# Three small operations of the expert stage in another order: a raw copy, its rounding, its low part

## The reference, cut to what matters

```python
for e in range(E):                                  # 4 experts, head width 64
    q = x @ wq[e]; k = x @ wk[e]; v = x @ wv[e]
    scores = scale * (q @ k.transpose(0, 2, 1))     # 576 x 576, causal
    a = np.exp(scores - scores.max(-1, keepdims=True))
    a /= a.sum(-1, keepdims=True) + 1e-09
    ye = a @ v @ wo[e]
    out += gate_of_the_two_chosen_experts * ye
```

## Time and profile before

| | us |
|---|---|
| median of 3 runs | 572.97 |
| lowest and highest | 572.64, 573.55 |
| the profiled execution, its own time | 571.48 |
| its span, first to last instruction | 569.7 |
| PE busy in the span | 544.0 (95%) |
| DVE, ACT, POOL busy | 339.4, 262.1, 233.4 |

### The profile page before, as it was taken

One profiled execution on the slowest core, in us unless ns is written; L12 is line 12 of the kernel. 1 busy time (PEld: TensorE's weight loads), 2 busy tenths in 40 slices (PEclk: granted clock), 3 DMA queues, 4 the chain that ended last, 5 costly groups with the idle time before them and its releaser, 6 DMA issues.

```text
span 569.7 us, 12200 instructions
## 1 busy us (share of the span) xinstructions
PE 544.0 (95%) x5008; PEld 483.7 (85%) x5008; DVE 339.4 (60%) x696; ACT 262.1 (46%) x656; POOL 233.4 (41%) x285
## 2 busy tenths in 40 slices
PE   6789899999999999999999999999999999999997
PEld 4779799999668989999867989999986799999765
DVE  3998968722577883851458687492156857440561
ACT  3657544223664632423475553332257463322574
POOL 5658655330454642341145364143035555230251
PEclk9889999999999999999999999999999999999999
DMA  8991202210003112111001220100000200000002
GB/s 296 350 319 42 75 13 62 75 33 1 2 1 124 35 44 55 52 46 32 1 2 54 74 75 1 32 1 1 1 2 2 84 2 1 0 1 2 2 1 84
DMA packets 8935, 29.62 MB, mean 52 GB/s; under 512 B 1200, under 2 KB 1200, under 8 KB 8880
## 3 DMA queue, kind: packets, MB, share of 16 engines
q1 hardware_dynamic: 6256, 24.12, 13.2%
q10 hardware_dynamic: 2624, 4.72, 2.6%
HBM read 24.12 MB, written 4.72 MB: 51 GB/s over the span
## 4 chain that ended last, share of the span: by engine, by line
PE 79%; DVE 9%; ACT 5%; POOL 4%; issue 3%; DMA 1%; POOLq 0%; ACTq 0%
PE MM L511 20%; PE MM L513 18%; PE MM L512 18%; PE SC L469 4%; PE OA L676 3%; PE SC L627 3%; PE TR L655 3%; PE OA L500 3%; PE TR L485 2%; ACT c_prob L840 2%; PE MM L621 2%; POOL prob L1263 1%; ACT c_probT L853 1%; DVE row_inv L1016 1%; DVE ring L1073 1%
## 5 line engine op out<-in xcount | busy, mean ns | idle before, releaser
L1292 POOL TENSOR_TENSOR k_lo<-ring,k_hi 128x288 fp32r<-128x288 f32 x64 | 54.4, 851 | 98.1 <-ACT k_hi L821 98.1
L1320 POOL TENSOR_SCALAR c_prob<-c_prob,c_inv,gates 128x512 f32<-128x512 f32 (+3 forms) x64 | 42.1, 666 | 109.9 <-DVE c_inv L1161 109.9
L511 PE MATMUL MM<-k_hi,wv_hi 128*128 128x288 f32 x256 | 76.2, 298 | 4.8 <-DVE ring L1079 2.6
L511 PE MATMUL MM<-act_hi,wk_hi 128*128 128x288 f32 x256 | 77.4, 302 | 0.0
L512 PE MATMUL MM<-k_lo,wv_hi 128*128 128x288 f32 x256 | 75.5, 295 | 0.0
L513 PE MATMUL MM<-k_hi,wv_lo 128*128 128x288 f32 x256 | 75.3, 294 | 0.0
L512 PE MATMUL MM<-act_lo,wk_hi 128*128 128x288 f32 x256 | 75.3, 294 | 0.0
L513 PE MATMUL MM<-act_hi,wk_lo 128*128 128x288 f32 x256 | 75.2, 294 | 0.0
L1093 DVE RECIPROCAL gate_r<-gate_r 128x288 f32<-128x288 f32 x32 | 62.5, 1953 | 1.1
L1073 DVE TENSOR_TENSOR ring<-ring 128x288 f32<-128x288 f32 x64 | 41.3, 653 | 25.6 <-ACT ring L834 25.3
L1048 DVE SCALAR_TENSOR_TENSOR mix<-xT,one_less,mix 128x288 f32<-128x288 f32 x64 | 51.1, 798 | 7.1 <-ACT mix L934 6.0
(11 more groups left out here) (173 smaller groups left out, 1372.2 us busy)
## 6 DMA issues: line engine op xcount, KB each, us to landing
qkT<-in_qk SPq DMA_DIRECT2D x16, 591.5 KB, 3.8
vn<-in_v SPq DMA_DIRECT2D x16, 432.0 KB, 3.8
out_x<-c_prob ACTq DMA_DIRECT2D x16, 224.0 KB, 2.5
raw_wk_lo<-in_w_k SPq DMA_DIRECT2D x4, 512.0 KB, 17.0
raw_wv_lo<-in_w_v SPq DMA_DIRECT2D x4, 512.0 KB, 19.1
raw_wr_lo<-in_w_r SPq DMA_DIRECT2D x2, 512.0 KB, 8.2
out_x<-c_prob ACTq DMA_DIRECT2D x4, 256.0 KB, 2.8
raw_cv_lo<-in_c_v SPq DMA_DIRECT2D x1, 520.0 KB, 18.0
```

The lines of the kernel that those rows point to most:

```text
L511: nc.tensor.matmul(dst, w2[0], x2[0], start=first, stop=False)
L1292: nc.gpsimd.tensor_tensor(lo, ring[:, ITEM[u] % RING, :], hi.bitcast(fp32), ALU.subtract)\
L1320: nc.gpsimd.tensor_scalar(prob_tile(u), prob_tile(u), c_inv[:, u:u + 1], gate, ALU.mult, ALU.mult).then_inc(c_prob, 1)
```

## The change

It has three parts, and a guard.

- ACT: the raw copy of the first pair's output moves from behind both exponentials of tile 7 to between them.
- ACT: for k = 7 the exponentials of tile 9 come ahead of the copies of tile 7, and the rounding of pair 0 comes behind these copies (`Y_SPLIT` one higher) and no longer ahead of them.
- DVE: the low part of pair 0 moves from between tile 8 and tile 9 to behind the statistics of tile 9.
- PE: `pe_out` of pair 0 now waits for the low part of pair 0 by a semaphore of its own.

```diff
-    Y_SPLIT = NT + 1
+    Y_SPLIT = NT + 2
...
                 if n < 2:
 
+                    pe.wait_ge(y_lo, b * EP + 1)
                     pe_out(pe, b, n, range(EP - 1))
...
             for k in range(PAIR_TILES):
+                last_exp = k == PAIR_TILES - 3
+                if last_exp:
+                    for u in TILE_UNITS[k + 2]:
+                        act_c_exp(act_, b, u)
                 for u in TILE_UNITS[k]:
                     act_c_turned(act_, b, u)
-                if k + 2 < PAIR_TILES:
+                if not last_exp and k + 2 < PAIR_TILES:
                     for u in TILE_UNITS[k + 2]:
                         act_c_exp(act_, b, u)
-                if k == NT:
-                    act_y_raw(act_, b)
+                        if (k, u) == (NT, TILE_UNITS[k + 2][0]):
+                            act_y_raw(act_, b)
                 if k == Y_SPLIT:
                     act_y_hi(act_, b, 0)
             act_y_hi(act_, b, EP - 1)
...
                 for u in TILE_UNITS[k]:
                     dve_c_stat(dve, b, u)
-                if k == Y_SPLIT + 2:
-                    dve_y_lo(dve, b, 0)
+            dve_y_lo(dve, b, 0)
             if ahead:
 
                 for j in pieces_behind(1, -2)[0:2]:
```

## The result

| | before | after |
|---|---|---|
| median of 8 runs each, us | 572.81 | 574.58 |
| lowest and highest | 571.34, 573.55 | 574.17, 576.73 |
| ratio, 95% interval | 1 | 1.0044 [1.003, 1.0057] |
| the profiled execution: time, span | 571.48, 569.7 | 574.66, 572.9 |

By the ratio the changed kernel is slower by 2.5 us (1.7 to 3.3 by the interval); the two medians lie 1.8 apart. The forecast was 575.2 us, +2.2, in a range of 573.3 to 576.4.

What follows compares the result with a forecast made beforehand. PE, 79% of the chain, was taken as the bound. Three batches at +0.63 (+1.9) and the last at +0.35 gave +2.2 us: 573.7 from the profiled 571.48, 575.2 from the median 572.97; range 573.3 to 576.4.

Steps and rivals of the forecast that it cites:

- Part 3: DVE: mixing starts 1.02 late behind the moved low part, so PE's second share comes 0.63 later in three batches.
- Part 2: ACT idles about 0.75 ahead of tile 9's exponentials, copies of tile 7 0.83 late; last batch's projection +0.35.
- Part 1: Raw copy on ACT: PE's product 0.56 earlier a batch, taken alone; tile 8's exponential 0.24 late.
- Part 4: PE's new wait for the first low part at the projection costs nothing, with 1.2 us to spare.
- A: Rival: ACT does not idle ahead of tile 9, each batch keeps 0.56, -2.2 us; 0.12 with half-way cases.
- B: Rival: rounding late but mixing short, 0.21 a batch and 0.2 in the last, +0.8 us; chance 0.18.
- C: Rival: mixing takes its old 3.00, tile 9's exponential 0.1 later still, +3.4 us; 0.10 together with D.
- D: Rival: raw copy waits for the first pair's products, PE's stall stays 0.72; 0.10 together with C.

Runs made afterwards that it cites:

- one_piece: The changed kernel with one mixing piece instead of two ahead of the second pair's low part on DVE; ratio 1.0005.
- best_two_pieces: rounding_last with two mixing pieces again ahead of the second low part; ratio 1.0026 against the kernel before.
- Copy_alone: The kernel before with only the raw copy moved between the two exponentials of tile 7; ratio 1.0020.
- late_copy: The changed kernel with the raw copy put back behind both exponentials of tile 7; ratio 1.0047 against the kernel before.
- guard_alone: The kernel before with only PE's new wait for the first low part added; ratio 1.0005.
- rounding_last: The changed kernel with ACT's old order for k = 7, one mixing piece ahead of the second low part, rounding one tile later; ratio 0.9949.
- before_one_piece: The kernel before with one mixing piece instead of two ahead of the second low part; ratio 0.9996.

## Why the prediction was right

**The waits.** Of the five signs that I named, all stood where I put them: the stall at 0.16, the wait ahead of tile 8's transposes at 0.84 (some 0.8), DVE's gap at 0.98 (about 1.0), PE's at 0.70 ahead of the second share in the first three batches only (0.7), and ACT's at 0.61 (0.75 was the distance from start to start). The clock times hit closely once the later start of 1.06 is taken off: exponentials of tile 9 at 163.27 (163.29 forecast), copies of tile 7 at 163.97 (163.99), mixing at 166.12 (166.16), second low part at 168.91 (168.94), second share at 169.71 (169.75).

**Part 3**, the largest term, was +0.63 and measured +0.59. That both pieces together take 2.78 rather than 3.00 was the right choice: 167.18 to 169.97 is 2.79. one_piece and best_two_pieces show that it is this queue. The long form of the mixing is not a wait to POOL's end and then a whole short one: POOL's low part ends at 169.39 (168.53 + 0.86), and the long instruction only 0.32 later (168.76 + 0.95), where a short one takes 0.52.

**Part 2**, the last batch: +0.35 forecast, +0.28 measured. Here the size is near and the reading was not right: I took it from the earlier trace rows that nothing waited ahead of the last transposes of that batch, but the row holds a wait of some 0.26 (0.70 less 0.44). The product of tile 7 came 0.48 late, as in the first batch, and most of that wait came back, so that the projection was 0.28 late. That my 0.35 fell near this is in part luck: I had taken it from 0.45 for the coarseness of the rows, not for this wait. In the first three batches the projection starts 0.14 earlier than before (9.21 against 9.35), where I had it about where it was.

**Part 1** was right in its working and loose in one sentence. I wrote that, taken alone, it is worth 0.56 a batch. Copy_alone measured a loss of 0.24: the price that I worked out, 0.24 at tile 8, goes through to the end of the kernel before, not only to that of the changed one. I had looked at the wait of 0.40 for POOL only as something that gives time back, and not as the sign that a second way was already the longer one. In the changed kernel itself part 1 costs 0.12 (late_copy), so the sum was not touched by it.

**Part 4** was right for this kernel: no wait of PE shows there, with 1.2 of cover (guard_alone tests the wait only where the cover is 3.7).

**The sum**, +2.2, against +2.0 in the marks and 2.5 (1.7 to 3.3) in the runs. Of the rivals, A would have needed tile 9's maximum by 162.3, and it started at 162.97 (164.03 less 1.06). B needed two short pieces; the long instruction of the second took 0.95. C needed 3.00 for the pieces, and they took 2.79. D fell with the stall at 0.16.

## What to carry to other kernels

Where a long queue is written out by hand, price a move by all ways that run through the stretch, not by the stall that it removes: a short wait elsewhere (here 0.40 for POOL) is the sign of a second way about as long. Such a wait can hide in a merged row, so compare the row's duration with the same work undisturbed (here 0.70 against 0.44). Put the work that waits for something late (a rounding, a low part) neither ahead of work that others need nor ahead of an unrelated long piece on an engine that must come back for the end of the stretch. And when an edit loses though its target wait went, look at what stands right behind the new waits: three small edits (ACT's old order for k = 7, the rounding one tile later, one mixing piece) made this loss of 2.5 us into a gain of 2.9.

## What the runs showed of the hardware that I had not expected

**A late store.** In ten of the twelve traces, not in those of before and before_one_piece, ACT waits once, in the first batch alone, for a store of the output to land. In rounding_last:

```profile
ACT c_prob L917 <- DMA out_x<-c_prob: 2.0, 1, 2.0
```
```profile
PE MM L511 <- ACT c_prob L917: 0.5, 1, 0.5
```

The chain has that store at 4.21 us from issue to landing, where the median of its 16 stores of 224 KB is 2.4. PE waits 0.5 by it. The stretch between the first two batches is longer than before's 126.79 in all ten: by 0.1 in the changed kernel, by 0.3 to 0.9 in the others. It doesn't follow the early projection, since guard_alone has 0.5 with its projection where it was. In later batches it never happens. With one trace of each kernel, it isn't shown whether it belongs to these kernels or to single executions, and why the store is slow was not tried.

**A cost of the one-piece edit.** All five kernels with one piece ahead of the second low part have 105.51 to 105.63 between the third and the last batch, where the two-piece kernels have 105.27 to 105.31. In before_one_piece PE's first matmul on the channel mix's own input (act_hi) starts late behind the last matmul of the gate's units (xr_hi):

```profile
457.97 0.29 PE L513 MATMUL MM<-xr_hi,wr_lo 128*128 128x288 f32 x1
458.30 0.37 PE L511 MATMUL MM<-act_hi,wk_hi 128*128 128x288 f32 x1
```

The step is 0.33 there and 0.13 in the kernel before (456.79 to 456.92). Seven pieces follow the second low part rather than six, and only in the last batch, which has no attention between its units, does PE come to them so early. POOL's times point to the same: its low parts of these pieces end at 458.43, and PE's second matmul, the first that reads one, starts at 458.51. In one_piece these are 457.69 and 457.77, in rounding_last 456.35 and 456.42, while in the kernel before POOL is done at 455.65 and PE comes at 457.05. That it is these pieces is still argued from the order and these times, not tested.
